# Attention, token mixing and two channel MLPs on one core: block sums in place in PSUM, the first inputs transposed during attention, and later low parts on GpSimd

## The chip, the cores and the metric

The kernel runs on one core of a Trainium2 chip. The metric is the device time in microseconds (us); smaller is better. TensorE is called PE here, VectorE DVE, ScalarE ACT, GpSimd POOL.

## The reference

Inputs are q, k and v of 2 batches x 8 heads x 768 rows x 64. Every row attends to a window of 31 neighbours and to 24 block summaries; then come a token-mixing MLP with a channel MLP, and a layer norm with a second channel MLP. All arithmetic is fp32.

```python
k_sum = k.reshape(B, H, nb, block, D).max(axis=3)
v_sum = v.reshape(B, H, nb, block, D).mean(axis=3)
scores_l_m = np.where(mask_l, scores_l, -1000000000.0)
...
a = np.exp(scores_all)
a = a / (np.sum(a, axis=-1, keepdims=True) + 1e-09)
x = np.matmul(a, v_all)                        # then (2, 768, 512)

h = np.maximum(xt @ w_tok1, 0.0) @ w_tok2      # 768 -> 256 -> 768
u = x + h.transpose(0, 2, 1)
x = u + np.maximum(u @ w_ch1, 0.0) @ w_ch2     # 512 -> 1536 -> 512

xn = (x - mu) / np.sqrt(var + 1e-06) * g_ln
out = x + np.maximum(xn @ w_ch1, 0.0) @ w_ch2  # 512 -> 2048 -> 512
```

## The kernel before

Each fp32 operand of a product is split into a high part (an fp32r copy, made by ACT) and a low part (the value minus its high part, made by DVE or POOL), and a product is three matmuls: low x high, high x low, high x high (`three`, L502).

**Attention** (L619 to L630 on PE) runs over 48 tiles n: scores, transposes of the probabilities, the product with the values. From tile 25 (`MIX0`) on, the token mixing of batch 0 goes between the tiles and ends at tile 42. Behind the loop PE runs the token mixing of batch 1, in which `first_batch` transposes batch 0's rows, eight times three 128x128 transposes; ACT copies each to `raw_in`, POOL makes four sums of blocks of `raw_in` (`t_in`, `sum_inputs`), ACT the high parts of seven inputs (`in_t`, `high_input`), DVE the low parts of two, POOL of the other five (`low_input`).

**The channel MLPs** are 28 pairs q of hidden slices in four groups g (batch 0 and 1 of the first MLP: 6 pairs each; batch 0 and 1 of the second: 8 each). A pair's up product is a 2x2 block product with seven multiplications instead of eight (Strassen-Winograd, `PRODUCTS`, L64). `up(q, i)` is six matmuls of 384 columns into one of two PSUM banks in turn (`up_bank`); between the seven products PE runs the twelve down units (three matmuls of 512 columns each) of the pair before, in the numbers of `DOWNS_AFTER`. The pairs' order on an engine is written out in its `pair`. Products 0 to 3 give p1, u2 and u3; products 4, 5 and 6, with u3 or u2 added by DVE (L1072, L1086, L1099), are three of the four blocks of the hidden layer, written to `c_raw` in SBUF. Of each block ACT makes the ReLU's high part (L828) and DVE the low part (L989). DVE also makes the low parts of the down weights (`low_down`) and of three of the seven up weights (`low_up`), POOL the sums of the up weights (`sum_weights`) and their low parts (`low_sums`, L422).

In 11 of the pairs PE also turns two or three batches (`turn_batch`, L593) of the next group's inputs behind its seven products (`BATCHES_AT`). A product or a batch may only start when the bank that it writes, the one of two products earlier, is free. POOL makes the sums of the next group's inputs in pairs 4, 10 and 17 (`T_AT`), and the last pair of a group (5, 11, 19) starts the next group's `in_t`. The second MLP's layer norm is made by DVE in the first two pairs of groups 1 and 2.

## Time and profile before

| | before |
|---|---|
| median of 3 runs | 644.25 us (643.85 to 644.62) |
| the profiled execution: its time | 643.52 us |
| the profiled execution: its span | 641.7 us |
| mean granted TensorE clock | 0.965 of full |

The span is what the trace covers; the execution's own time is 1.8 us longer. Busy time is what an engine's instructions took; an idle time in brackets in a timeline row is the time that the engine had nothing to run just before the row, and the arrow names what ended it. PEclk is the granted TensorE clock of a stretch, 1.00 being 2.4 GHz and 0.50 being 1.2 GHz.

### The profile page before, as it was taken

The numbers are of one execution on the slowest core, as the hardware profiler recorded it, in microseconds if no ns is written. First come the engines' busy times: TensorE is split into PE (matmuls) and PEld (weight loads), VectorE is DVE, ScalarE is ACT, GpSimd is POOL, SyncE is SP. The second block draws the span as 40 slices with busy tenths as digits, with TensorE's granted clock in tenths as the row PEclk, the third lists the DMA queues.
The fourth block names the chain that finished last, engine by engine and source line by source line (L and its number), as shares of the span: only waits on it lengthen the run. The fifth ranks groups of instructions, "written<-read, shape, count | busy, mean of one in ns | idle before, by whom it ended". The sixth has DMA issues, their size and how long they took to land.

```text
span 641.7 us, 8274 instructions
## 1 busy us (share of the span) xinstructions
PE 592.1 (92%) x2976; PEld 512.1 (80%) x2976; DVE 356.0 (55%) x675; ACT 244.5 (38%) x450; POOL 291.2 (45%) x267
## 2 busy tenths in 40 slices
PE   5989999858999989799989979999899989999998
PEld 2777888647888878688878868888799868989896
DVE  6577665335544548784463878444635664444435
ACT  3577664422333234244423423333324323333321
POOL 5365653274444457534454843444561843333300
PEclk9899999887999989899998979999989989999999
DMA  8977722000311011112110111111101111111302
GB/s 232 243 221 203 213 61 78 0 1 5 121 54 56 30 65 66 65 51 82 65 42 25 66 65 66 67 65 66 65 2 66 66 66 65 66 66 65 132 1 99
DMA packets 24896, 50.34 MB, mean 78 GB/s; under 512 B 7596, under 2 KB 7832, under 8 KB 24856
## 3 DMA queue, kind: packets, MB, share of 16 engines
q1 hardware_dynamic: 24304, 49.37, 23.6%
q10 hardware_dynamic: 552, 0.44, 0.3%
q8 instruction: 24, 0.39, 0.2%
q14 instruction: 16, 0.13, 0.1%
HBM read 46.07 MB, written 3.15 MB: 77 GB/s over the span
## 4 chain that ended last, share of the span: by engine, by line
PE 70%; DVE 13%; POOL 6%; issue 4%; ACT 4%; DMA 2%; SPq 1%; DVEq 0%; POOLq 0%; ACTq 0%
PE bank L500 67%; DVE hidden L989 5%; POOL in_t L453 3%; DVE down_w L914 2%; PE bank L593 2%; DMA tok_stage<-w_tok 1%; ACT hidden L828 1%; ACT in_t L806 1%; DMA k_sb<-k_w 1%; DVE neg_scores L932 1%; DVE c_raw L1086 1%; DVE c_raw L1072 1%; ACT probs L755 1%; DVE k_sb L920 1%; PE bank L535 0%
## 5 line engine op out<-in xcount | busy, mean ns | idle before, releaser
L500 PE MATMUL bank<-down_w,hidden 128*128 128x512 f32 x1008 | 277.1, 404 | 5.3 <-issue 3.1
L500 PEld LDWEIGHTS bank<-down_w,hidden 128*128 128x128 f32 x1008 | 190.0, 193 | 34.0 <-issue 6.6
L500 PE MATMUL bank<-in_t,up_even 128*128 128x384 f32 x588 | 121.9, 344 | 10.7 <-ACT p L834 6.0
L500 PE MATMUL bank<-in_t,up_odd 128*128 128x384 f32 x588 | 123.2, 346 | 7.5 <-DVE c_raw L1086 7.5
L500 PEld LDWEIGHTS bank<-in_t,up_even 128*128 128x128 f32 x588 | 107.4, 192 | 20.5 <-ACT p L834 6.4
L500 PEld LDWEIGHTS bank<-in_t,up_odd 128*128 128x128 f32 x588 | 108.4, 193 | 17.8 <-issue 8.7
L828 ACT ACTIVATE hidden<-c_raw 128x384 fp32r<-128x384 f32 x84 | 44.1, 525 | 176.9 <-DVE c_raw L1072 85.1
L989 DVE SCALAR_TENSOR_TENSOR hidden<-c_raw,hidden 128x384 fp32r<-128x384 f32 x84 | 75.9, 903 | 39.4 <-ACT hidden L828 39.4
L422 POOL TENSOR_TENSOR up_even<-sums_up,up_even 128x1024 fp32r<-128x1024 f32 x14 | 33.6, 2401 | 120.5 <-ACT up_even L818 120.4
L422 POOL TENSOR_TENSOR up_odd<-sums_up,up_odd 128x1024 fp32r<-128x1024 f32 x14 | 33.5, 2392 | 98.5 <-ACT up_odd L818 98.5
L1042 DVE TENSOR_TENSOR u<-bank,p 128x384 f32<-128x384 f32 x28 | 15.6, 557 | 88.3 <-PE bank L500 80.5
L828 ACT ACTIVATE hidden<-bank 128x384 fp32r<-128x384 f32 x28 | 13.8, 492 | 90.9 <-PE bank L500 90.9
L500 PE MATMUL bank<-k_sb,q_sb 128*128 128x364 f32 x96 | 39.1, 493 | 5.6 <-POOL k_sb L371 3.1
L755 ACT ACTIVATE probs<-neg_scores,neg_max 128x182 f32<-128x182 f32 x96 | 37.6, 441 | 13.8 <-DVE neg_max L932 13.2
L932 DVE CUSTOM_DVE_ANT_0 neg_scores<-bank,mask_sb 128x182 f32<-128x182 f32 x96 | 29.3, 342 | 22.8 <-PE bank L500 20.9
L914 DVE TENSOR_TENSOR down_w<-raw_down,down_w 128x1024 fp32r<-128x1024 f32 x28 | 39.5, 1412 | 0.0
L989 DVE SCALAR_TENSOR_TENSOR hidden<-bank,hidden 128x384 fp32r<-128x384 f32 x28 | 15.6, 556 | 34.8 <-ACT hidden L828 34.8
L764 ACT COPY probs_t<-bank 128x384 f32<-128x384 f32 x48 | 22.7, 473 | 30.2 <-PE bank L535 30.0
L1072 DVE TENSOR_TENSOR c_raw<-bank,u 128x384 f32<-128x384 f32 x28 | 15.6, 557 | 29.5 <-PE bank L500 29.2
L414 POOL TENSOR_TENSOR sums_up<-raw_up 128x256 f32<-128x256 f32 x28 | 28.4, 1015 | 2.2
L824 ACT CAST down_w<-raw_down 128x1024 fp32r<-128x1024 f32 x28 | 28.9, 1034 | 0.0
L1059 DVE TENSOR_TENSOR u<-bank,p 128x384 f32<-128x384 f32 x28 | 15.6, 556 | 24.1 <-PE bank L500 24.1
(89 smaller groups left out, 758.4 us busy)
## 6 DMA issues: line engine op xcount, KB each, us to landing
raw_up<-w_ch SPq DMA_DIRECT2D x28, 512.0 KB, 4.3
raw_down<-w_ch SPq DMA_DIRECT2D x28, 512.0 KB, 3.5
k_sb<-k_w SPq DMA_DIRECT2D x16, 273.0 KB, 4.7
v_own<-v_w SPq DMA_DIRECT2D x8, 390.0 KB, 3.1
q_sb<-q_t SPq DMA_DIRECT2D x8, 384.0 KB, 5.7
v_turned<-v_t SPq DMA_DIRECT2D x8, 384.0 KB, 4.3
out<-natural SPq DMA_DIRECT2D x12, 256.0 KB, 3.1
tok_stage<-w_tok SPq DMA_DIRECT2D x4, 384.0 KB, 5.3
```

Source lines behind the costliest of these rows:

```text
L414: tt(sums_up[:, S3], raw[:, A11], raw[:, A21], ALU.subtract).then_inc(up_sum, 1)
L422: nc.gpsimd.tensor_tensor(w[:, 1, 3:7, :], sums_up[:], w[:, 0, 3:7, :].bitcast(F32), ALU.subtract).then_inc(sums_low, 1)
L453: nc.gpsimd.tensor_tensor(in_t[:, i, 1], src, in_t[:, i, 0].bitcast(F32), ALU.subtract).then_inc(in_low_pool, 1)
L500: return nc.tensor.matmul(dst, lhs, rhs, start=start, stop=stop, skip_group_check=True)
L755: nc.scalar.activation(probs[:, n % 2, h * NK:(h + 1) * NK], neg_scores[:, n % 2, h, :], ACT.Exp, bias=neg_max[:, n % 2, h:h + 1], scale=- ...
L764: nc.scalar.copy(probs_t[:, n % 2, :], turn_bank[n % 2][:, 0:3 * P]).then_inc(turned_copied, 1)
L824: nc.scalar.copy(down_w[:, q % 2, :, 0, :], raw_down[:, q % 2]).then_inc(down_high, 1)
L828: nc.scalar.activation(hidden[:, q % 2, f, 0, h * HN:(h + 1) * HN], src, ACT.Relu).then_inc(hid_high, 1)
L914: return nc.vector.tensor_tensor(dst, src, high.bitcast(F32), ALU.subtract)
L932: nc.vector.tensor_tensor_reduce(neg_scores[:, n % 2, h, :], score_bank[n % 3][:, h * NK:(h + 1) * NK], mask_sb[:, kind, (1 - h) * NSUM:(1 ...
L989: nc.vector.scalar_tensor_tensor(out=hidden[:, q % 2, f, 1, at], in0=src, scalar=0.0, in1=hidden[:, q % 2, f, 0, at].bitcast(F32), op0=ALU ...
L1072: nc.vector.tensor_tensor(c_raw[:, 0], product_bank(q, 4)[:, 0:HN], u3[:], ALU.add).then_inc(c_made, 1)
```

## The change

**Block sums.** DVE adds u3 or u2 to products 4, 5 and 6 in the PSUM bank where they stand, and ACT and DVE make the high and low part from the bank. `c_raw` is gone. The bank is free for the next product when the low part is made (`hid_low`), where before it was free when the sum was in `c_raw` (`c_made`). Product 6 no longer accumulates onto product 4; instead DVE adds product 4 to u2 in an instruction of its own. `low_down` moves from between the sum and the low part of block 2 to behind u3; on ACT `high_down` moves ahead of block 1 and `high_sums(q + 1)` behind it.

**First inputs.** Batch 0's 24 transposes are made tile by tile (`first_tile`: four 128x128 transposes into `mix_bank`) in tiles 43 to 47 of attention and once behind the loop; ACT copies 512 columns each time. The four sums and seven low parts of group 0 are DVE's. The up weights of pair 1 are split in pair 0 and no longer in tiles 43 to 45. The first two loads of down weights wait for the last attention tile.

**Later inputs.** The seven low parts of groups 1 to 3 are all POOL's; DVE has none.

The core of the diff:

```diff
@@ DVE, pair(q)
-                dve.wait_ge(u_made, 2 * q + 2)
-                nc.vector.tensor_tensor(c_raw[:, 0], product_bank(q, 4)[:, 0:HN], u3[:], ALU.add).then_inc(c_made, 1)
-                low_hidden(q, 1, c_raw[:, 0])
+                dve.wait_ge(u_made, 3 * q + 2)
+                nc.vector.tensor_tensor(u2[:], product_bank(q, 4)[:, 0:HN], u2[:], ALU.add).then_inc(u_made, 1)
+                add_c(q, 0, 4, u3)
+                low_hidden(q, 1, product_bank(q, 4)[:, 0:HN])
...
+            def add_c(q, k, i, u):
+                c = product_bank(q, i)[:, 0:HN]
+                dve.wait_ge(up_done, 7 * q + i + 1)
+                dve.wait_ge(u_made, 3 * q + 3)
+                nc.vector.tensor_tensor(c, c, u[:], ALU.add).then_inc(c_made, 1)
@@ PE, up and pair(q)
-                                 lambda s: in_t[:, b, s, c, :], i not in (2, 3, 6) and c == 0, c == 1)
+                                 lambda s: in_t[:, b, s, c, :], i not in (2, 3) and c == 0, c == 1)
...
                     if i == 6:
-                        pe.wait_ge(c_made, 3 * q + 1)
+                        pe.wait_ge(hid_low, 4 * q + 2)
...
                     if b < 2:
-                        pe.wait_ge(c_made, 3 * q + 2 + b)
+                        pe.wait_ge(hid_low, 4 * q + 3 + b)
@@ PE, attention
+            def first_tile(t):
+                if t == 0:
+                    pe.wait_ge(u_done, NT)
+                else:
+                    pe.wait_ge(first_copied, t)
+                for c in range(C):
+                    last = nc.tensor.transpose(mix_bank[:, c * P:(c + 1) * P], natural[:, t, c * P:(c + 1) * P],
+                                               ident[:])
+                last.then_inc(first_turned, 1)
...
+                if n >= TURN0:
+                    first_tile(n - TURN0)
@@ ACT, pair(q)
-                if q and q + 1 < NQ:
-                    high_sums(q + 1)
...
                 act.wait_ge(c_made, 3 * q + 1)
-                high_hidden(q, 1, c_raw[:, 0])
-                high_down(q)
+                high_hidden(q, 1, product_bank(q, 4)[:, 0:HN])
+                if making:
+                    high_sums(q + 1)
```

Where the instructions stand, in three places. The first is an ordinary pair on DVE (pair 4 before and after): `up_odd` and `down_w` rows are the low parts of weights, `hidden` rows the low parts of the hidden layer. Before:

```order
L1042 TENSOR_TENSOR u<-bank,p 128x384 [waits p1_copied,up_done]
L914 TENSOR_TENSOR up_odd<-raw_up,up_odd 128x768 [waits up_high]
L989 SCALAR_TENSOR_TENSOR hidden<-bank,hidden 128x384 [waits hid_high]
L1059 TENSOR_TENSOR u<-bank,p 128x384 [waits up_done]
L1072 TENSOR_TENSOR c_raw<-bank,u 128x384 [waits u_made,up_done]
L989 SCALAR_TENSOR_TENSOR hidden<-c_raw,hidden 128x384 [waits hid_high]
L1086 TENSOR_TENSOR c_raw<-bank,u 128x384 [waits up_done]
L914 TENSOR_TENSOR down_w<-raw_down,down_w 128x2x512 [waits down_high]
L989 SCALAR_TENSOR_TENSOR hidden<-c_raw,hidden 128x384 [waits hid_high]
L1099 TENSOR_TENSOR c_raw<-bank,u 128x384 [waits up_done]
L989 SCALAR_TENSOR_TENSOR hidden<-c_raw,hidden 128x384 [waits hid_high]
```

Of the change:

```order
L1061 TENSOR_TENSOR u<-bank,p 128x384 [waits p1_copied,up_done]
L923 TENSOR_TENSOR up_odd<-raw_up,up_odd 128x768 [waits up_high]
L1003 SCALAR_TENSOR_TENSOR hidden<-bank,hidden 128x384 [waits hid_high]
L1080 TENSOR_TENSOR u<-bank,p 128x384 [waits up_done]
L923 TENSOR_TENSOR down_w<-raw_down,down_w 128x2x512 [waits down_high]
L1093 TENSOR_TENSOR u<-bank,u 128x384 [waits u_made,up_done]
L1011 TENSOR_TENSOR bank<-bank,u 128x384 [waits u_made,up_done]
L1003 SCALAR_TENSOR_TENSOR hidden<-bank,hidden 128x384 [waits hid_high]
L1011 TENSOR_TENSOR bank<-bank,u 128x384 [waits u_made,up_done]
L1003 SCALAR_TENSOR_TENSOR hidden<-bank,hidden 128x384 [waits hid_high]
L1011 TENSOR_TENSOR bank<-bank,u 128x384 [waits u_made,up_done]
L1003 SCALAR_TENSOR_TENSOR hidden<-bank,hidden 128x384 [waits hid_high]
```

The low part of `down_w` has moved ahead of the three block sums, the sums write `bank`, every `hidden` row reads `bank`, and one addition (L1093) is new between the product and the first block sum.

The second place is DVE between the end of attention and pair 0: `x_split` is the split of batch 1 for the token mixing, `h_tok` its hidden layer, `t_in` and `in_t` the sums and low parts of the channel MLP's first inputs. Before:

```order
L914 TENSOR_TENSOR up_odd<-raw_up,up_odd 128x768 [waits up_high]
L914 TENSOR_TENSOR x_split<-natural,x_split 128x3x128 [waits x_high_end]
L941 TENSOR_SCALAR den<-bank 128x6 [waits pv_done]
L943 RECIPROCAL den<-den 128x6 [waits den_step]
L945 TENSOR_TENSOR natural<-bank,den 128x3x128 [waits den_step]
L914 TENSOR_TENSOR x_split<-natural,x_split 128x3x128 [waits x_high_end]
L962 SCALAR_TENSOR_TENSOR h_tok<-bank,h_tok 128x512 [waits h_high] x2
L914 TENSOR_TENSOR in_t<-raw_in,in_t 128x768 [waits in_high]
L914 TENSOR_TENSOR in_t<-t_in,in_t 128x768 [waits in_high]
```

Of the change:

```order
L923 TENSOR_TENSOR x_split<-natural,x_split 128x3x128 [waits x_high_end]
L983 TENSOR_TENSOR t_in<-raw_in 128x768 [waits first_copied]
L983 TENSOR_TENSOR t_in<-raw_in,t_in 128x768 [waits first_sum]
L923 TENSOR_TENSOR in_t<-raw_in,in_t 128x768 [waits in_high]
L983 TENSOR_TENSOR t_in<-raw_in 128x768 [waits first_sum]
L923 TENSOR_TENSOR in_t<-t_in,in_t 128x768 [waits in_high]
L971 SCALAR_TENSOR_TENSOR h_tok<-bank,h_tok 128x512 [waits h_high]
L923 TENSOR_TENSOR in_t<-raw_in,in_t 128x768 [waits in_high]
L971 SCALAR_TENSOR_TENSOR h_tok<-bank,h_tok 128x512 [waits h_high]
L923 TENSOR_TENSOR in_t<-t_in,in_t 128x768 [waits in_high]
L983 TENSOR_TENSOR t_in<-raw_in,t_in 128x768 [waits first_sum]
```

The low part of `up_odd` no longer stands ahead of the first `x_split` row; four sums and two more low parts have come to DVE ahead of pair 0, two of them ahead of the first `h_tok` row.

The third place is POOL at the first change of group, from `low_sums` of pair 6 (`up_even`) to the first sum of pair 7's up weights. Before:

```order
L422 TENSOR_TENSOR up_even<-sums_up,up_even 128x1024 [waits up_high,sums_made]
L453 TENSOR_TENSOR in_t<-raw_in,in_t 128x768 [waits in_high,sums_low]
L453 TENSOR_TENSOR in_t<-t_in,in_t 128x768 [waits in_high,in_low_pool] x3
L453 TENSOR_TENSOR in_t<-raw_in,in_t 128x768 [waits in_high,in_low_pool]
L410 TENSOR_TENSOR sums_up<-raw_up 128x256 [waits sums_low,ld_up1,in_low_pool]
```

Of the change:

```order
L424 TENSOR_TENSOR up_even<-sums_up,up_even 128x1024 [waits up_high,sums_made]
L447 TENSOR_TENSOR in_t<-raw_in,in_t 128x768 [waits in_high,sums_low]
L447 TENSOR_TENSOR in_t<-t_in,in_t 128x768 [waits in_high,in_low_pool]
L447 TENSOR_TENSOR in_t<-raw_in,in_t 128x768 [waits in_high,in_low_pool]
L447 TENSOR_TENSOR in_t<-t_in,in_t 128x768 [waits in_high,in_low_pool] x3
L447 TENSOR_TENSOR in_t<-raw_in,in_t 128x768 [waits in_high,in_low_pool]
L412 TENSOR_TENSOR sums_up<-raw_up 128x256 [waits sums_low,ld_up1,in_low_pool]
```

Seven low parts of inputs stand where five stood.

## Rows read from the trace of the kernel before

**Rows 1.** The page, part 1: engine, busy us, share, instructions.

```profile
PE 592.1 (92%) x2976; PEld 512.1 (80%) x2976; DVE 356.0 (55%) x675; ACT 244.5 (38%) x450; POOL 291.2 (45%) x267
```

**Rows 2.** Windows: stretch, length, each engine's busy us, PEclk, DMA share, GB/s.

```profile
113.20:159.50 46.30, 33.57 (x150) 28.71 (x149) 17.30 (x24) 14.55 (x26) 22.33 (x14) 0.85 0.00 0
...
175.90:208.80 32.90, 32.90 (x170) 29.30 (x169) 14.94 (x22) 11.82 (x20) 13.24 (x10) 1.00 0.18 63
...
245.50:272.70 27.20, 22.68 (x103) 19.42 (x102) 21.36 (x27) 8.88 (x14) 18.59 (x14) 0.94 0.22 78
...
332.40:343.30 10.90, 7.85 (x27) 6.48 (x26) 4.46 (x4) 2.76 (x5) 7.71 (x7) 0.69 0.26 96
...
117.00:120.30 3.30, 3.30 (x9) 2.55 (x8) 0.00 (x0) 0.00 (x0) 0.00 (x0) 0.50 0.00 0
```

**Rows 3.** Timeline, 112 to 160 us: start, us, engine, instruction, [idle before <-releaser].

```profile
114.18 2.45 DVE L914 TENSOR_TENSOR x_split<-natural,x_split 128x384 fp32r<-128x384 f32 x1 [0.62 <-ACT x_split L776]
...
116.69 3.91 PE L500 MATMUL bank<-x_split,tok_w 128*128 128x512 f32 x9 [2.96 <-DVE x_split L914]
...
122.81 0.56 DVE L914 TENSOR_TENSOR x_split<-natural,x_split 128x384 fp32r<-128x384 f32 x1 [0.58 <-ACT x_split L776]
...
132.77 0.95 DVE L914 TENSOR_TENSOR in_t<-raw_in,in_t 128x768 fp32r<-128x768 f32 x1
...
133.87 2.12 PE L500 MATMUL bank<-in_t,up_even 128*128 128x384 f32 x6 [3.77 <-DVE in_t L914]
...
146.54 2.29 PE L500 MATMUL bank<-in_t,up_even 128*128 128x384 f32 x6 [6.00 <-ACT p L834]
...
159.54 1.23 PE L500 MATMUL bank<-in_t,up_odd 128*128 128x384 f32 x6
```

**Rows 4.** Timeline of an ordinary pair, 185 to 193 us.

```profile
185.62 0.56 DVE L1072 TENSOR_TENSOR c_raw<-bank,u 128x384 f32<-128x384 f32 x1 [1.18 <-PE bank L500]
...
186.22 0.53 ACT L828 ACTIVATE hidden<-c_raw 128x384 fp32r<-128x384 f32 x1 [2.64 <-DVE c_raw L1072]
...
187.84 1.28 DVE L914 TENSOR_TENSOR down_w<-raw_down,down_w 128x1024 fp32r<-128x1024 f32 x1
...
187.86 1.21 PE L500 MATMUL bank<-in_t,up_even 128*128 128x384 f32 x6
...
190.66 0.55 PE L593 MATMUL bank<-ident,natural 128*128 128x128 f32 x3
...
192.44 1.22 PE L500 MATMUL bank<-in_t,up_odd 128*128 128x384 f32 x6
```

**Rows 5.** Timeline of pair 4, where GpSimd sums the next inputs.

```profile
223.07 2.67 POOL L441 TENSOR_TENSOR t_in<-raw_in 128x768 f32<-128x768 f32 x1
...
224.00 2.15 DVE L989 SCALAR_TENSOR_TENSOR hidden<-c_raw,hidden 128x384 fp32r<-128x384 f32 x1
...
226.68 0.90 PE L593 MATMUL bank<-ident,natural 128*128 128x128 f32 x3 [3.06 <-DVE c_raw L1099]
...
229.78 1.21 PE L500 MATMUL bank<-in_t,up_odd 128*128 128x384 f32 x6
```

**Rows 6.** Timeline around the first change of group.

```profile
249.36 3.79 POOL L453 TENSOR_TENSOR in_t<-t_in,in_t 128x768 fp32r<-128x768 f32 x2 [0.56 <-ACT in_t L806]
...
258.97 1.05 ACT L818 CAST up_odd<-sums_up 128x1024 fp32r<-128x1024 f32 x1 [6.11 <-POOL sums_up L416]
...
264.77 1.28 PE L500 MATMUL bank<-in_t,up_odd 128*128 128x384 f32 x6 [2.73 <-DVE c_raw L1086]
```

**Rows 7.** Instructions of line 989 by operands: duration ns min/median/max, first and last start.

```profile
L989 DVE SCALAR_TENSOR_TENSOR hidden<-c_raw,hidden x84: 543/584/2498, 156.0 to 630.4; 128x384 fp32r<-128x384 f32 x84
L989 DVE SCALAR_TENSOR_TENSOR hidden<-bank,hidden x28: 544/558/560, 149.4 to 621.1; 128x384 fp32r<-128x384 f32 x28
```

**Rows 8.** Waits of TensorE: waiter, releaser, us in total, times, longest us.

```profile
PE bank L593 <- DVE c_raw L1099: 9.1, 3, 3.1
PE bank L500 <- DVE c_raw L1086: 8.4, 5, 2.7
```

More of the change, by code:

```diff
@@ L477, in _ @@
                     sum_weights(1)
[L478 to L482 removed]
+            for q in range(NQ):
                 g, j = group_of(q)
[L484 removed]
+                making = q + 1 < NQ
+                if g and j == 0:
                     for i in range(LATE_IN, 7):
                         low_input(g, i)
[L487 removed]
+                if making and q:
                     sum_weights(q + 1)
+                if making:
                     low_sums(q + 1)
@@ L1047, in pair @@
                     row_stats(g - 1, 5)
[L1048 removed]
+                if q + 1 < NQ:
                     low_up(q + 1)
```

247 lines of the change are left out of this document (122 added, 125 removed).

## The prediction

> **What bounds the kernel now.** First the page: TensorE (PE) is busy for 592.1 us, 92% of the span [rows 1]. So the kernel is bound by PE, and what can be won is of two kinds: time in which PE has nothing to run, and time in which it runs at half clock. The windows show where these lie. In two ordinary pairs (175.9 to 208.8 us) PE is busy for 32.90 of 32.90 us at PEclk 1.00: a pair takes 16.45 us and has no slack to give. From 113.2 to 159.5 us, the hand-over from attention to the first pair of the channel MLP, it is busy for 33.57 of 46.30 us at 0.85; at the first change of group (245.5 to 272.7) for 22.68 of 27.20 us at 0.94 [rows 2].
>
> Then the timeline, for what ends these waits. In the hand-over PE idles 2.96 us until DVE has a low part of `x_split` (2.45 us long, though the same instruction takes 0.56 us at 122.81), 3.77 us for the first low part of `in_t`, and 6.00 us for ACT's copy of p1, which stands on ACT behind the high parts that wait for POOL's four sums [rows 3]. In pair 4 it idles 3.06 us: POOL runs a sum of 2.67 us, DVE's low part of the hidden layer takes 2.15 us beside it, so the sum behind it (L1099) comes late, and the batch at 226.68 waits for that [rows 5]. The trace has the same picture twice more, in pairs 10 and 17: three waits of L593 for L1099 make 9.1 us [rows 8]. By operands, the low part from `c_raw` takes 543 to 2,498 ns, the one from a bank 544 to 560 ns in all 28 cases [rows 7]: with two SBUF operands DVE can be held up by POOL, with one it is not here. At a change of group, five waits for line 1086 cost 8.4 us [rows 8].
>
> After each long idle time PE is granted 1.2 GHz for a while: 9 matmuls at 116.69 take 3.91 us, with PEclk 0.50 [rows 2, 3]; in 332.4 to 343.3 the mean is 0.69 [rows 2]. From the ordinary 1.78 us between the second batch and the next pair (190.66 to 192.44) it becomes 3.10 us behind the wait of pair 4 (226.68 to 229.78), 1.3 us more [rows 4, 5].
>
> **The change, part by part.** I work in the times of the profiled execution (span 641.7 us).
>
> *Hand-over.* The low part of pair 1's up weights on DVE and POOL's low sums leave the end of attention, so `x_split` has its 0.56 us and the wait of 2.96 us goes: PE would be ready at 116.69 - 2.96 = 113.73. Four tiles of four transposes come ahead of it. Three transposes fill a row of 0.55 us with their latency [rows 4]; back to back I take 0.11 us each, so 1.76 us, and ACT's and DVE's split is ready by then. The matmuls start at about 115.4. From 116.69 to the first matmul of pair 1 at 159.54 [rows 3] there are 42.85 us. Without the waits of 3.77 and 6.00 that is 33.1 of work. PEclk 0.85 over 46.30 us means some 14 us at half clock; about 10 of them are busy after 116.69 and would run in half the time, so 28.1 at full clock. 24 transposes leave (2.6), two tiles remain (0.9): 26.4. New waits: the last tile waits for ACT's copy of the one before (0.75, a copy of 512 columns estimated at 0.6); PE then reaches the second layer of batch 1's token mixing about 1.0 us before DVE has its low part, since five sums and low parts at 0.95 us [rows 3] stand ahead of the first `h_tok` row and one between the two; and pair 1 waits about 0.9 us for the bank of product 5 in pair 0, where DVE has extra work. That gives 115.4 + 26.4 + 2.7 = 144.5; I take 144.9. **-14.7 us.** ACT's p1 is then behind one high part that waits for no POOL sum. The loads of down weights start with the end of attention, some 17 us before use.
>
> *Pairs 4, 10 and 17.* `hidden` rows have one SBUF operand and no longer stand beside POOL's sums with two; `low_down`, which still has two, now comes before those sums, since POOL's `low_sums` and with them `sum_inputs` come later. The three waits, 9.1 us [rows 8], go, and the half clock behind them: 1.3 us for the first as above, 1.5 for the third, and up to 2.7 for the second (0.69 over 10.90 us is 6.8 us at half clock, of which some 5.5 busy) [rows 2, 5]. 9.1 + 5.5: **-14.6 us.**
>
> *Every pair: the bank is held longer.* Product 6 now waits until the sum, the high part and the low part of block 0 are made in the bank of product 4. Product 4 is done at 185.62, product 6 starts at 187.86 [rows 4]. New chain: product 4 added to u2 0.56, sum 0.56, high part 0.53 [rows 4], low part 0.56 [rows 7], four hand-overs of 0.04 (ACT starts 0.04 behind the sum's end, rows of pair 2): 2.37, so 187.99. About +0.1 us. Blocks 1 and 2 follow one after the other, because DVE waits for ACT between a sum and its low part: 1.55 to 1.6 us each. The second batch waits for the low part of block 2: 187.99 + 3.1 = 191.1 instead of 190.66 [rows 4], **+0.45 us in each of the 11 pairs with batches**. Against it stands that `low_down` (1.28 us at 187.84 [rows 4]) no longer lies between these steps; it now lies behind u3, where DVE idled 1.18 us before 185.62 [rows 4]; overlapping its neighbours' ends a little, it is just covered. If that cover is missed, the whole chain is late by as much. In the some 13 ordinary pairs without batches only the 0.1 remains: the next pair begins two down units later. 11 x 0.45 + 13 x 0.1 = **+6.2 us**.
>
> No row has DVE writing to PSUM from PSUM. Lower bound: the sum from a bank to SBUF, 0.56 us; upper: the slowest row of the same width, 2.15 us beside POOL [rows 5], which would not hold here as the sum has one SBUF operand. I take 0.56, as it is the same operation, and widen the range by 0.1 us for each of three sums in the 11 pairs, 3 us.
>
> The Trainium skill speaks against reading the bank: in "VectorE: DVE Perf Modes", section on the TRN2 errata, an instruction of VectorE with a PSUM source has a fixed part of 120 cycles at 0.96 GHz, one with an SBUF source 58, so 65 ns more for each low part, or an estimated 2 us more over 11 chains of three. The trace does not agree: 558 ns from a bank against 543 at least and 584 in the median from `c_raw` [rows 7]. The sum above goes by the trace.
>
> *Changes of group.* Before, the first costs 4.5 us of idle time and, at a mean of 0.94 over 27.2 us, 1.6 us of clock [rows 2]; with short waits for L1086 in the pair behind it (part of the 8.4 us [rows 8]) I count 6.8 us, and take the other two as equal. After, `low_sums` stands behind the high part of block 0 and ends about 6 us later, and POOL has seven low parts of 1.9 us (3.79 for two [rows 6]) behind it, of which the new group's first product needs one. I find the next group's first product about 2.5 us late; product 6 of that pair 1.6 us late, as `low_down` meets POOL's low parts and add-outs stand ahead of the block sums; and the sums of pair 7's weights end about 5 us later than the 258.97 of before, where ACT waited 6.11 us for them [rows 6]. That wait no longer stands ahead of block 0's high part but ahead of block 1's, and I find 0.75 us for it and 0.4 for the product behind, where it cost 2.73 us and more [rows 6]. With 0.5 us for short waits that is 5.8 us, against 6.8: **-1.0 us each, -3**; half clock behind the wait of 2.5 us would add some 1.4 each.
>
> Sum: 641.7 - 14.7 - 14.6 + 6.2 - 3.0 = 615.6 us of span. The execution's own time is 1.8 us above its span, 617.4, and the median of the runs is 0.7 above this execution: **618 us**.
>
> **The rivals.**
> - *The hand-over gives half* (0.15): DVE now has 11 sums and low parts there at 0.95 us each, 10.5 us; if ACT and DVE hand over less well than one after the other, or PE drops to half clock once more, 7 us are lost again: 625 us. For it: PE's largest waits were of this kind. Against: POOL is idle then, so nothing holds DVE up.
> - *POOL alone is too slow at the changes of group* (0.12): the low parts meet DVE's two-operand rows at 2.5 us instead of 1.9, and PE is granted half clock behind each wait. 3 to 4 us for each: 628 us. For it: POOL already had the critical chain there. Against: two fewer DVE rows with two SBUF operands.
> - *The waits of pairs 4, 10 and 17 stay* (0.08): the change doesn't do what it says, because another row with two SBUF operands, `low_down`, is held by POOL's sums. Three waits of 3 us and the clock come back: 632 us. Against: by the order they no longer meet.
> - *Slower than before* (0.05): holding the bank is what decides. The chain has three sums in place; in 11 pairs all three lie before the second batch, in the others one or two before a product. If a sum in place takes x longer, that is about 60x over the program. From x = 0.45 us on (1.0 us a sum) it eats the gain of 26; at 0.5 us, 648 us. For it: no row shows this form. Against: every narrow bank row is within 0.56.
> - The forecast has 0.60; its own range is 612 to 625 us.
>
> **How the numbers follow.** Below: a hand-over with fewer of the new waits and changes of group without half clock, 609. Above, up to 631, which takes in the first two rivals and leaves the last two, and the forecast's own tails, outside. A measurement of this kernel can tell about 0.2% (1.3 us). Slower: the last rival, 0.05, and 0.01 for several at once; same 0.02; faster the rest.
>
> **What would show it.** In the changed kernel's trace: the first matmul of pair 1 at about 145 us; no wait of 3 us in pairs 4, 10, 17, but one of about 0.4 us in front of each second batch, ended by a `hidden` row; `bank<-bank,u` at about 0.56 us; `hidden` rows never over 0.6 us; in the first change of group a wait of 2 to 3 us for POOL's `in_t`. The prediction is wrong if sums in place are longer, if the second batch waits for over 1 us, or if the half clock returns in the hand-over.

## The result, and the profile after

The changed kernel takes 620.25 us (median of 4 runs, 618.54 to 621.6) against 644.05 us (643.22 to 644.62): ratio 0.963, 95% interval 0.9597 to 0.9663. The forecast was 618 us, range 609 to 631. The profiled execution took 621.6 us, its span is 619.8.

The page of the changed kernel, its first part and its largest DVE groups (columns as in [rows 1]; then line, engine, operation, out<-in, shapes, count | busy us, mean ns | idle before it in us and what ended it):

```profile
PE 589.4 (95%) x2976; PEld 499.5 (81%) x2976; DVE 339.7 (55%) x706; ACT 243.2 (39%) x448; POOL 267.8 (43%) x264
...
L1003 DVE SCALAR_TENSOR_TENSOR hidden<-bank,hidden 128x384 fp32r<-128x384 f32 x112 | 62.5, 558 | 82.3 <-ACT hidden L835 82.3
L1011 DVE TENSOR_TENSOR bank<-bank,u 128x384 f32<-128x384 f32 x84 | 46.9, 559 | 2.9
```

PE's share rose from 92 to 95% [rows 1]: PE stands idle for 30.4 us of the span where it stood idle for 49.6, so nearly all of the gain is idle time. The sum in place, for which no row stood before, takes 559 ns, and no low part is held any more: 112 of them average 558 ns, where 84 from `c_raw` reached 2,498 [rows 7].

Windows of the changed kernel: the hand-over, most of two ordinary pairs (3 and 4), and the stretch behind a change of group.

```profile
112.50:143.80 31.30, 29.00 (x158) 25.16 (x156) 23.20 (x37) 15.77 (x27) 1.84 (x1) 1.00 0.24 84
176.90:210.10 33.20, 33.05 (x165) 28.41 (x163) 14.76 (x24) 11.66 (x20) 9.98 (x10) 1.00 0.17 64
230.80:234.20 3.40, 3.40 (x11) 2.93 (x10) 0.00 (x0) 1.88 (x3) 3.24 (x3) 0.50 0.00 0
```

The hand-over of [rows 2], 46.30 us at 0.85, has become 31.30 us at 1.00. The ordinary pairs, which had no idle time before, now have a little. Behind attention, half clock is left only where GpSimd (POOL) is late, behind the first and third change of group. The timeline of the changed kernel: hand-over, ordinary pair, first change of group.

```profile
114.29 0.56 DVE L923 TENSOR_TENSOR x_split<-natural,x_split 128x384 fp32r<-128x384 f32 x1 [0.87 <-ACT x_split L770]
...
119.52 0.63 PE L586 MATMUL bank<-ident,natural 128*128 128x128 f32 x4 [0.77 <-ACT raw_in L780]
...
128.45 1.62 PE L492 MATMUL bank<-h_tok,tok_w 128*128 128x512 f32 x6 [1.07 <-DVE h_tok L971]
...
187.65 0.56 DVE L1093 TENSOR_TENSOR u<-bank,u 128x384 f32<-128x384 f32 x1
188.15 1.23 PE L492 MATMUL bank<-in_t,up_odd 128*128 128x384 f32 x6
188.31 0.57 DVE L1011 TENSOR_TENSOR bank<-bank,u 128x384 f32<-128x384 f32 x1
189.44 0.56 DVE L1003 SCALAR_TENSOR_TENSOR hidden<-bank,hidden 128x384 fp32r<-128x384 f32 x1 [0.56 <-ACT hidden L835]
190.05 1.32 PE L492 MATMUL bank<-in_t,up_odd 128*128 128x384 f32 x6
192.61 0.56 DVE L1003 SCALAR_TENSOR_TENSOR hidden<-bank,hidden 128x384 fp32r<-128x384 f32 x1 [0.56 <-ACT hidden L835]
193.22 0.55 PE L595 MATMUL bank<-ident,natural 128*128 128x128 f32 x3
...
225.94 2.41 POOL L424 TENSOR_TENSOR up_even<-sums_up,up_even 128x1024 fp32r<-128x1024 f32 x1 [4.52 <-ACT up_even L825]
228.43 1.81 POOL L447 TENSOR_TENSOR in_t<-raw_in,in_t 128x768 fp32r<-128x768 f32 x1
230.38 1.90 PE L492 MATMUL bank<-in_t,up_even 128*128 128x384 f32 x6 [2.15 <-POOL in_t L447]
...
241.09 2.34 DVE L923 TENSOR_TENSOR down_w<-raw_down,down_w 128x1024 fp32r<-128x1024 f32 x1
```

Three things answer to the rows of before. The low part of `x_split` takes 0.56 us where it took 2.45, and the waits of 2.96, 3.77 and 6.00 us [rows 3] are now 0.77 and 1.07. The chain in the bank (187.65 to 190.05) is the one that the prediction wrote out; product 6 (190.05) and the pair's second batch (193.22) start just behind the low part that frees their bank. And the new group's first product waits 2.15 us for POOL, which first makes a low part of weights (225.94) although it had stood idle for 4.52 us.

### The profile page after: what moved, and what is told of

It is laid out like the page before. It is cut to its first block, busy times and chain, and to the rows that moved or that the text cites. A ratio compares the mean times of both kernels' runs of the same rounds, so it can differ in the third digit from the quotient of the medians.

```text
span 619.8 us, 8385 instructions
## 1 busy us (share of the span) xinstructions
PE 589.4 (95%) x2976; PEld 499.5 (81%) x2976; DVE 339.7 (55%) x706; ACT 243.2 (39%) x448; POOL 267.8 (43%) x264
## 4 chain that ended last, share of the span: by engine, by line
PE 66%; DVE 14%; ACT 7%; issue 6%; POOL 3%; DMA 2%; SPq 1%; DVEq 0%; POOLq 0%; ACTq 0%
PE bank L492 63%; DVE bank L1011 4%; ACT hidden L835 4%; POOL in_t L447 3%; DVE hidden L1003 2%; DVE u L1093 2%; PE bank L595 1%; DMA tok_stage<-w_tok 1%; DVE to_turn L1048 1%; DMA k_sb<-k_w 1%; DVE in_t L923 1%; ACT in_t L813 1%; DVE neg_scores L941 1%; DVE k_sb L929 1%; ACT probs L749 1%
## 5 line engine op out<-in xcount | busy, mean ns | idle before, releaser
L492 PE MATMUL bank<-down_w,hidden 128*128 128x512 f32 x1008 | 273.4, 399 | 0.0
L492 PEld LDWEIGHTS bank<-down_w,hidden 128*128 128x128 f32 x1008 | 187.4, 190 | 27.2
L835 ACT ACTIVATE hidden<-bank 128x384 fp32r<-128x384 f32 x112 | 55.1, 492 | 258.0 <-DVE bank L1011 158.3
L492 PEld LDWEIGHTS bank<-in_t,up_even 128*128 128x128 f32 x588 | 104.7, 189 | 26.4 <-issue 10.5
L492 PEld LDWEIGHTS bank<-in_t,up_odd 128*128 128x128 f32 x588 | 104.4, 188 | 16.9 <-DVE hidden L1003 6.1
L1003 DVE SCALAR_TENSOR_TENSOR hidden<-bank,hidden 128x384 fp32r<-128x384 f32 x112 | 62.5, 558 | 82.3 <-ACT hidden L835 82.3
L424 POOL TENSOR_TENSOR up_odd<-sums_up,up_odd 128x1024 fp32r<-128x1024 f32 x14 | 33.6, 2398 | 135.4 <-ACT up_odd L825 135.4
L424 POOL TENSOR_TENSOR up_even<-sums_up,up_even 128x1024 fp32r<-128x1024 f32 x14 | 34.2, 2441 | 124.0 <-ACT up_even L825 123.9
L1011 DVE TENSOR_TENSOR bank<-bank,u 128x384 f32<-128x384 f32 x84 | 46.9, 559 | 2.9
L749 ACT ACTIVATE probs<-neg_scores,neg_max 128x182 f32<-128x182 f32 x96 | 37.7, 441 | 15.9 <-DVE neg_max L941 15.3
L843 ACT COPY p<-bank 128x384 f32<-128x384 f32 x28 | 13.4, 480 | 36.5 <-PE bank L492 36.4
L492 PE MATMUL bank<-v_own,probs_t 128*128 128x65 f32 x192 | 26.7, 261 | 0.0
L412 POOL TENSOR_TENSOR sums_up<-raw_up 128x256 f32<-128x256 f32 x28 | 24.1, 860 | 4.0 <-POOL up_odd L424 1.9
```

What stands on the lines that cost most here:

```text
L412: tt(sums_up[:, S1], raw[:, A21], raw[:, A22], ALU.add).then_inc(up_sum, 1)
L424: nc.gpsimd.tensor_tensor(w[:, 1, 3:7, :], sums_up[:], w[:, 0, 3:7, :].bitcast(F32), ALU.subtract).then_inc(sums_low, 1)
L492: return nc.tensor.matmul(dst, lhs, rhs, start=start, stop=stop, skip_group_check=True)
L749: nc.scalar.activation(probs[:, n % 2, h * NK:(h + 1) * NK], neg_scores[:, n % 2, h, :], ACT.Exp, bias=neg_max[:, n % 2, h:h + 1], scale=- ...
L835: nc.scalar.activation(hidden[:, q % 2, f, 0, h * HN:(h + 1) * HN], src, ACT.Relu).then_inc(hid_high, 1)
L1003: nc.vector.scalar_tensor_tensor(out=hidden[:, q % 2, f, 1, at], in0=src, scalar=0.0, in1=hidden[:, q % 2, f, 0, at].bitcast(F32), op0=ALU ...
```

## The experiments

Medians are of 4 to 6 runs each, the range or the 95% interval in brackets; the kernel before took 643.37 us beside the first four, 644.53 beside the next four, 643.55, 644.65 and 644.3 beside the last. Times of a pair run from its first matmul to the next pair's, in the timeline. A profile is of one execution: the first matmul of pair 0 lies anywhere between 125.75 and 129.07 us in the thirteen kernels with the new attention part, which is the same in all, so two spans can differ by 3 us without a cause in the pairs. Blocks 1 to 3 of the hidden layer are those of products 4, 5 and 6, as in the section on the change; the prediction counts them from 0.

### The parts of the change

**The hand-over alone**: before, with the attention part of the change (`first_tile`, group 0's sums and low parts on DVE, down loads later); `c_raw`, the old order and the later groups as before.

```diff
+                if n >= TURN0:
+                    first_tile(n - TURN0)
```

> The kernel before with the hand-over part alone: batch 0's transposes in attention tiles 43 to 47, DVE's four sums and seven low parts for group 0, pair 1's up weights split in pair 0; block sums in c_raw and the split of later low parts (two DVE, five GpSimd) as before. By my theory the parts add up, and this one gives what the first matmul of pair 1 shows (159.5 to 143.8 us): 15.7 us less than before, 628 us, with the waits of 3 us in pairs 4, 10 and 17 and at the changes of group where they were. The rival, that part of the 15.7 us is only borrowed and given back in the pairs behind (weights split later, loads later), gives 632 us or more.

629.21 us, ratio 0.9769 (0.9738 to 0.9799): -14.2 us. The three waits for L1014, the sum for the second batch, are all there (9.0 us in total). So the hand-over is worth 14 us by itself, close to the 15.7 of the theory, little of it is given back in the pairs behind (the rival's 632 us), and the waits of pairs 4, 10 and 17 are another matter.

**The later low parts on POOL, too**: the seven low parts of groups 1 to 3, otherwise as the kernel above.

```diff
-                    for i in range(DVE_IN, LATE_IN):
+                    for i in range(LATE_IN):
                         low_input(g + 1, i)
```

> As e1, and all seven low parts of groups 1 to 3 on GpSimd; sums in c_raw, old order of the weights' work. By my theory GpSimd carries the chain at each change of group, and two more low parts of 1.9 us in front of its sums of weights cost 2 to 4 us each time: 634 to 640 us. The rival, that GpSimd has room and the move costs nothing, gives 628 us.

633.44 us (629.01 to 636.27), ratio 0.983 (0.9776 to 0.9884): about 4 us slower than without this part, and just below the forecast 634 to 640. The two intervals touch, so that it costs by itself is likely, not shown. Pairs 6, 12 and 20 take 21.1, 21.2 and 20.5 us, where they took 19.3, 19.3 and 18.7; pairs 7, 13 and 21 give back 0.9, 0.3 and 2.7.

**The order, but not the bank**: the changed kernel with the block sums written to `c_raw` again, the bank free at the sum, and product 6 accumulated onto product 4 again, without the addition to u2.

```diff
-                nc.vector.tensor_tensor(c, c, u[:], ALU.add).then_inc(c_made, 1)
+                nc.vector.tensor_tensor(c_raw[:, k], c, u[:], ALU.add).then_inc(c_made, 1)
```

> The changed kernel, but block sums go to c_raw and the bank is free at the sum, as before; everything else (hand-over, GpSimd's low parts, the new places of low_down, high_down and high_sums) as changed. Theory: the second SBUF operand is what cost the 3 us waits, so low parts from c_raw again take up to 2.5 us beside GpSimd's sums, and waits of 2 to 3 us stand in or behind pairs 4, 10 and 17, while the ordinary pairs with batches fall from 17.05 back to about 16.5 us: the two about cancel, 618 to 623 us. Rival: the new order alone takes the waits away, then this kernel is faster than the changed one by the price of the held bank, about 9 us: 611 us.

622.51 us (622.08 to 624.29), ratio 0.9679 (0.9658 to 0.9701). The sum is inside the range, but its reasons were wrong: pairs with batches take 17.0 us, not 16.5, and pairs 4, 10 and 17 take 17.0, 17.0 and 17.1, without any wait of 3 us. The timeline of this kernel, of an ordinary pair, of pair 4 (208.21) and behind the first change of group:

```profile
190.56 2.39 POOL L425 TENSOR_TENSOR up_even<-sums_up,up_even 128x1024 fp32r<-128x1024 f32 x1 [11.04 <-ACT up_even L826]
...
191.22 2.15 DVE L1004 SCALAR_TENSOR_TENSOR hidden<-c_raw,hidden 128x384 fp32r<-128x384 f32 x1 [0.59 <-ACT hidden L836]
...
193.29 0.55 DVE L1012 TENSOR_TENSOR c_raw<-bank,u 128x384 f32<-128x384 f32 x1
...
193.89 0.55 PE L596 MATMUL bank<-ident,natural 128*128 128x128 f32 x3 [0.37 <-DVE c_raw L1012]
...
208.21 2.16 DVE L1004 SCALAR_TENSOR_TENSOR hidden<-c_raw,hidden 128x384 fp32r<-128x384 f32 x1 [0.59 <-ACT hidden L836]
...
248.71 2.37 POOL L425 TENSOR_TENSOR up_odd<-sums_up,up_odd 128x1024 fp32r<-128x1024 f32 x1 [1.23 <-ACT up_odd L826]
249.13 2.36 DVE L1004 SCALAR_TENSOR_TENSOR hidden<-c_raw,hidden 128x384 fp32r<-128x384 f32 x1 [0.59 <-ACT hidden L836]
...
251.59 2.88 PE L493 MATMUL bank<-down_w,hidden 128*128 128x512 f32 x6 [1.61 <-issue]
```

With two SBUF operands the low part is still held, now beside POOL's low part of the weights: 1116 ns in the mean of 84. In an ordinary pair PE waits 0.37 us for it in front of the second batch, and the pair takes as long (17.0 us) as with the held bank of the changed kernel. Behind the changes of group it costs a wait and half clock: pairs 7, 13 and 21 take 19.3, 21.7 and 19.7 us, against 16.6, 16.7 and 16.0; pairs 6, 12 and 20 give back 1.4, 2.2 and 1.2.

**The bank, but not the order**: the changed kernel with `low_down` between sum and low part of block 2, and `high_sums`, `high_down` and two of each later group's `high_input` on ACT where they were.

```diff
-                low_down(q)
...
                 add_c(q, 1, 5, u3)
+                low_down(q)
                 low_hidden(q, 2, product_bank(q, 5)[:, 0:HN])
```

> The changed kernel with sums in place, but low_down between the sum and the low part of block 2, high_sums ahead of block 0's high part and high_down behind it, as before. Theory: the order matters where GpSimd is busy: low_down (two SBUF operands) is blocked beside GpSimd's sums in pairs 4, 10 and 17, ACT's high parts wait for the sums of weights at a change of group, and in every pair 1.3 us of low_down lie in the chain that holds the bank, so a batch pair takes about 18 us: 635 us or more. Rival: in place sums alone bring the gain and the order is worth under 3 us: 623 us at most.

627.2 us (626.18 to 628.27), ratio 0.9747 (0.9725 to 0.9769), between the two theories (635 or more, 623 at most). Pairs with batches take 17.7 us, pairs 4, 10 and 17 take 19.0, 18.9 and 19.0: in pair 4 `low_down` takes 2.67 us at 211.17, beside POOL's sums of inputs, and the two batches behind wait 1.50 and 0.34 us. The four medians with the hand-over and POOL's low parts together:

| | `c_raw` | in the bank |
|---|---|---|
| old order | 633.4 | 627.2 |
| new order | 622.5 | 620.3 |

The order is worth 10.9 us with `c_raw` and 6.9 us with the bank; the bank is worth 6.2 and 2.3 us. The second is hardly more than the intervals, and the changed kernel was timed apart from the other three, with 644.05 us for the kernel before beside it. The waits of 3 us of [rows 5] go by either, but with the bank alone pairs 4, 10 and 17 stay 1.3 us longer than their neighbours.

### What the change left

**One low part back on DVE**: that of each later group's first product.

```diff
+                if ending:
+                    low_first(0, g + 1)
```

> The changed kernel with the first low part of each later group's inputs (product 0's own) back on VectorE, ahead of the sum of block 2 in the last pair of the group before; the other six stay on GpSimd. In the changed kernel product 0 of groups 1 to 3 waits 2.15, 2.15 and 2.16 us for that low part on GpSimd (L447), and TensorE runs at half clock for 3.4 us after two of the three waits, which costs about 1.7 us each. Theory A (the waits come from GpSimd alone, which takes the low part only behind its own low part of the sums' weights, L424): the three waits go, of each some 0.3 to 0.5 us comes back because the sums of blocks 2 and 3 stand 0.95 us later on VectorE; with the half clock gone 620.3 - 3 x 1.7 - 2 x 1.7 = about 612, range 610 to 615. Rival B (VectorE's low part reads two SBUF operands while GpSimd is at L424 and is held to its end, as low_down was for 2.34 us): it takes about 2.4 us instead of 0.95, blocks 2 and 3 are late by as much, product 0 or 1 waits 1 to 2 us for hidden; 616 to 620.

614.92 us (614.3 to 615.62), ratio 0.9541 (0.9522 to 0.956): 5.3 us less than the changed kernel. That is in theory A's range (610 to 615), at its upper end. DVE's low part starts at 225.93, 0.57 us before POOL's low part of the weights, and takes 0.95 us; PE stands idle for 0.11 us in front of product 0, and no half clock is left between 25 and 610 us. So giving POOL this low part, in the order of the change, did not pay.

**POOL's first two low parts ahead of its low part of the weights**, in the last pair of each group, into the 4.52 us in which it stood idle.

```diff
+                if ending:
+                    low_input(g + 1, 0)
+                    low_input(g + 1, 1)
                 if making:
                     low_sums(q + 1)
```

> The changed kernel with GpSimd's first two low parts of the next group's inputs put ahead of the low part of the sums' weights (L424) in the last pair of each group; nothing else moves. In the changed kernel GpSimd sits idle there from 221.4 to 225.9 us, while the high parts of these two inputs are ready at 220.4 and 221.1. Theory A: the waits of 2.15, 2.15 and 2.16 us at product 0 and the half clock behind two of them (about 1.7 us each) go, and nothing else comes: 620.3 - 6.5 - 3.4 = 610.4, range 609 to 613. Rival B: the two low parts last past 225.9 (2.4 us each beside VectorE), L424 ends 1 us later and product 1 or 3, which need the sums' low parts, wait in its place: 613 to 617. Rival C (waits of a pair are covered by another one right behind): over 617.

612.01 us (611.16 to 614.47), ratio 0.9506 (0.9484 to 0.9528), -8.2 us: three waits and two stretches of half clock, as theory A has it. It is the order on POOL, not its speed, that made them. Behind it, product 6 of pair 6 waits 1.57 us for `hidden`, 1.46 in the changed kernel.

**One down unit from the end of each pair to just ahead of product 6.**

```diff
-DOWNS_AFTER = {0: (2, 2, 2, 2, 1, 1, 2), 2: (2, 2, 1, 1, 1, 1, 1, 1, 2), 3: (2, 1, 1, 1, 1, 1, 1, 1, 1, 2)}
+DOWNS_AFTER = {0: (2, 2, 2, 2, 1, 2, 1), 2: (2, 2, 1, 1, 1, 2, 1, 1, 1), 3: (2, 1, 1, 1, 1, 2, 1, 1, 1, 1)}
```

> The changed kernel with one down unit (0.70 us of TensorE) moved from the end of each pair to just ahead of product 6, in all pairs but none of the sums changed. In the changed kernel product 6 starts 0.14 us late in the ordinary pairs and batch 2 about 0.29 us late, both behind hidden L1003, since the product's bank is held until its low part is read. Theory A (the in-place sums hold a bank too long by just that): pairs with batches fall from 17.05 to about 16.6, pairs without from 16.0 to about 15.85, and the changes of group gain some of their waits of 0.9 to 1.5 us for hidden: 620.3 - 14 x 0.43 - 8 x 0.14 - 2 = about 611, range 609 to 614. Rival B (the +0.6 and +0.3 us per pair are matmuls that run slower, not waits): 617 to 620. Rival C (with one unit less at the end of a pair the next pair's products 0 and 1 wait for the last low part or for the copied batch): 620 or more.

616.92 us (614.3 to 619.66), ratio 0.9571 (0.9547 to 0.9595): -3.3 us by the medians, just below B's range (617 to 620) and far from A's (609 to 614). Pairs without batches fall from 16.0 to 15.75 us, those with batches from 17.05 to 16.7: the first had waited for the bank only; in the others the second batch still starts up to 0.2 us late. The changes of group gained little: at the first, product 6 of pair 6 waits 0.42 us instead of 1.46, but pair 7's first product, one unit earlier now, 1.66 instead of 0.16.

**Both.**

> The two edits before together (GpSimd's two low parts ahead, one down unit ahead of product 6). If both theories A hold and the gains add: 620.3 - 9.9 - 9 = about 602, range 600 to 606. If the second of them is nothing: 610 to 612. If neither: 617 to 621.

607.46 us (606.17 to 608.02), ratio 0.9417 (0.9397 to 0.9437): the gains add, 12.8 us against 8.2 and 3.3. The forecast of 600 to 606 had taken theory A's larger gain for the down unit, and is missed.

**Both, with `c_raw`.** The same edit as for the order without the bank.

> The kernel of the two edits together (607.46 us), with the block sums written to c_raw in SBUF again and the bank free at the sum; the order, GpSimd's share and the unit ahead of product 6 stay. Theory A (a low part that reads c_raw beside a running GpSimd operation is held for as long as that one lasts, as at 249.13 in the run with c_raw and the new order, 2.36 us instead of 0.56, which made TensorE wait 1.61 us and then run 3.4 us at half clock): behind each change of group a held low part costs 1.6 to 3.3 us, the bank free earlier gives back a part of the waits of 1.2 and 0.9 us for hidden in the pair before; 607.5 + 3 x 2.5 - 3 x 1.5 = about 610, range 608 to 613. Rival B (with the order right the sums in place earn nothing, and the bank is held for nothing): 603 to 607.

606.14 us (604.31 to 607.74), ratio 0.9401 (0.9364 to 0.9437). Rival B: once the order is right, on POOL too and with the unit ahead of product 6, sums in place earn nothing in total that can be told. By pairs both theories are half right. With batches `c_raw` gives 16.4 us against 16.7; pairs 6, 12 and 20 take 17.0, 16.7 and 15.7 against 18.3, 18.3 and 16.6; pairs 7, 13 and 21 take 20.2, 20.0 and 18.3 against 16.6, 16.7 and 15.9.

**Both, with `low_down` later** in the first pair of groups 1 to 3, behind the low part of block 1.

```diff
+                if not opening:
+                    low_down(q)
...
                 low_hidden(q, 1, product_bank(q, 4)[:, 0:HN])
+                if opening:
+                    low_down(q)
```

> The kernel of the two edits together (607.46 us), with the low part of the down weights (low_down, two SBUF operands) in the first pair of groups 1 to 3 moved from between u3 and the sums to behind the low part of block 1; all other pairs as before. In that kernel it takes 2.80 us at 237.05, beside GpSimd's last low part of the inputs (L447 at 236.92), against 1.22 us in an ordinary pair, and product 6 then waits 1.22 us and the next pair's product 0 another 0.86 us, both for hidden. Theory A (these waits are the held low_down, 2.8 us ahead of the chain of sums): in each of the three pairs 1.2 to 2.1 us go; 607.5 - 3 x 1.5 = about 603, range 601.5 to 605. Rival B (the output's additions and row statistics, 2 x 1.28 us per product in that chain, are enough to keep it late, or low_down is held by GpSimd at its new place too): 605.5 to 608.

606.95 us (605.14 to 608.81), ratio 0.9416 (0.9381 to 0.945): no gain that can be told, rival B. The timeline of this kernel in pair 6:

```profile
243.23 1.22 DVE L927 TENSOR_TENSOR down_w<-raw_down,down_w 128x1024 fp32r<-128x1024 f32 x1
243.29 1.75 POOL L418 TENSOR_TENSOR sums_up<-raw_up,sums_up 128x256 f32<-128x256 f32 x1
...
245.08 1.05 ACT L829 CAST up_odd<-sums_up 128x1024 fp32r<-128x1024 f32 x1 [2.35 <-POOL sums_up L418]
245.56 0.55 DVE L1015 TENSOR_TENSOR bank<-bank,u 128x384 f32<-128x384 f32 x1
...
246.14 0.49 ACT L839 ACTIVATE hidden<-bank 128x384 fp32r<-128x384 f32 x1
...
247.37 1.30 PE L496 MATMUL bank<-in_t,up_odd 128*128 128x384 f32 x6 [1.54 <-DVE hidden L1007]
```

`low_down` now takes 1.22 us, but it started first, so POOL's sum was held (1.75 us instead of 0.74), and ACT waits for that sum in front of its cast. The wait of PE before product 6 is gone, the one before pair 7 is 1.54 us where it was 0.86. Two chains end together there: ACT's cast is done at 246.13, and block 2's sum, which stands on DVE behind `low_down`, an addition of the output and a row's statistics, at 246.11. So either would have kept the high part of block 2 (246.14) as late, and this run does not tell them apart.

**One block in place, in six pairs**: both edits, `c_raw`, and the sum of block 2 in the bank in the last pair of groups 0 to 2 and the first of groups 1 to 3.

```diff
+        def sum_at(q, k):
+            return product_bank(q, 5)[:, 0:HN] if k == 1 and in_place(q) else c_raw[:, k]
```

> The kernel of the two edits with c_raw in SBUF (606.14 us), with one block sum in place in PSUM again: that of block 2 (product 5's bank), in the last pair of groups 0 to 2 and the first pair of groups 1 to 3 alone, six of 84 sums. With c_raw its low part starts beside GpSimd's low part of the sums' weights (L425) there and takes 2.76 and 2.44 us instead of 0.56; TensorE then waits 1.01 and 2.58 us in front of the down matmuls, and 3.4 us of half clock stand behind the second at two of three places. In the other pairs c_raw lets go of the bank at the sum: 16.4 and 15.8 us a pair, where the sums in place take 16.7 and 15.8. Theory A (a sum in place pays only where its low part meets a long operation on GpSimd, and costs a late batch elsewhere): pairs 7, 13 and 21 fall from 20.2, 20.0 and 18.3 to some 17.0, 16.9 and 16.0, the pairs ahead of them lose up to 0.4: 606.1 - 8.6 + 1 = about 598, range 596.5 to 600. Rival B (something else of these pairs, so the low parts of blocks 1 and 3 from c_raw, or the held bank, is late in its place): 601 to 607.

604.17 us (602.54 to 605.49), ratio 0.9373 (0.9343 to 0.9404), 2 us less than with `c_raw` alone, within the intervals. Pairs 7, 13 and 21 fall to 17.4, 17.4 and 15.9, but pairs 6, 12 and 20 rise to 18.5, 18.3 and 16.8: rival B, another row is late. The timeline of this kernel:

```profile
237.28 2.73 POOL L456 TENSOR_TENSOR in_t<-raw_in,in_t 128x768 fp32r<-128x768 f32 x1
...
243.49 1.04 ACT L840 CAST up_odd<-sums_up 128x1024 fp32r<-128x1024 f32 x1 [2.99 <-POOL sums_up L427]
244.44 0.48 ACT L850 ACTIVATE hidden<-bank 128x384 fp32r<-128x384 f32 x1
...
244.96 0.56 DVE L1018 SCALAR_TENSOR_TENSOR hidden<-bank,hidden 128x384 fp32r<-128x384 f32 x1 [2.06 <-ACT hidden L850]
...
245.66 2.16 PE L505 MATMUL bank<-in_t,up_odd 128*128 128x384 f32 x6 [2.55 <-DVE hidden L1018]
```

Block 2's sum was in the bank at 242.90, but ACT stood for 2.99 us in front of a cast that waits for POOL's sums of weights, and its high part of block 2 is queued behind. POOL is late with the sums: the low parts of inputs lie ahead of them, the last one (237.28) held to 2.73 us by `low_down`.

**That cast one block later**, in the first pair of groups 1 to 3, with block 3 of the six pairs in the bank too.

```diff
-                if making:
+                if making and not opening:
                     high_sums(q + 1)
...
                 high_hidden(q, 2, sum_at(q, 1))
+                if making and opening:
+                    high_sums(q + 1)
```

> The mixed kernel (604.17 us) with ScalarE's high part of the sums' weights (L840, high_sums) in the first pair of groups 1 to 3 moved behind the high part of block 2, and block 3's sum of the same six pairs in place too, since GpSimd's low part of the sums' weights will then lie beside its low part. In the mixed kernel ScalarE stands 2.99 us in front of that cast, until GpSimd, late with the last low part of the inputs (237.28 to 240.01), has made the sums at 243.46; the high part of block 2 stands behind it in ScalarE's order, and the next pair's product 0 waits 2.55 us, with 3.4 us of half clock behind two of the three. Theory A (the wait is ScalarE's order, behind GpSimd's queue): each of the three waits goes but for 0.3 us, the half clock too; 604.2 - 3 x 2.2 - 2 x 1.7 = about 594, and 596 if the sums' low part is late for product 1 once; range 593 to 598. Rival B (the output's additions and row statistics between the sums on VectorE, 1.28 us per product, make blocks 2 and 3 nearly as late, as in the kernel with all sums in place): 599 to 603.

597.84 us (596.06 to 598.66), ratio 0.9288 (0.9253 to 0.9322): theory A, at the upper end of its range. The timeline of this kernel, the same place:

```profile
241.01 0.49 ACT L852 ACTIVATE hidden<-bank 128x384 fp32r<-128x384 f32 x1 [2.44 <-DVE bank L1031]
...
241.58 1.05 ACT L842 CAST up_odd<-sums_up 128x1024 fp32r<-128x1024 f32 x1
242.24 1.30 PE L505 MATMUL bank<-in_t,up_odd 128*128 128x384 f32 x6 [0.64 <-DVE hidden L1023]
...
245.22 0.97 PE L505 MATMUL bank<-in_t,up_odd 128*128 128x384 f32 x4 [0.28 <-POOL up_odd L433]
```

The wait of 2.55 us is 0.64, no stretch between 25 and 590 us is at half clock, and a change of group (pairs 5 to 7) takes 49.0 us, where it took 54.4 in the changed kernel and 54.6 before. This version beats both kernels: 22 us below the change, 46 below before. The run moved two things at once, the cast and block 3's sum; the waits of ACT that went are the cast's, but how the 6.3 us divide between the two was not measured.

## Why the prediction was right, step by step

By the profiled executions the span fell from 641.7 to 619.8 us, -21.9; forecast was -26.1. The terms, from the pairs' starts in both timelines:

| term | forecast | measured |
|---|---|---|
| hand-over | -14.7 | -15.7 |
| pairs 4, 10, 17, with the half clock behind them | -14.6 | -14.9 |
| bank held, 11 pairs with batches | +5.0 | +7.5 |
| the same, pairs without | +1.3 | +2.3 |
| changes of group | -3.0 | -2.3 |
| last matmul to the end | 0 | +1.2 |

The second row takes pairs 4, 10, 17 and 18 and 1.2 us of pair 11, which was at half clock before; what the held bank costs in these pairs is in the third and fourth. The first row holds whatever the two executions differ by in attention, and the start of pair 0 alone varies by 3 us between them, so its 1.0 us beyond the forecast tells nothing.

- **Hand-over: right.** The first matmul of pair 1 is at 143.8 us (forecast 144.9, 0.4 of it added to the sum without a reason; 159.54 before [rows 3]). The three new waits, forecast 0.75, 1.0 and 0.9, are 0.77, 1.07 and 0.47, and no half clock is left. The run with this part alone gives 14.2 of the 23.8 us between the medians.
- **Pairs 4, 10 and 17: size right, reason too narrow.** The three waits of 9.1 us [rows 8] are gone and the pairs take 17.0, 17.0 and 17.1. The step said that the low part's single SBUF operand does this, together with the place of `low_down`. The run with `c_raw` in the new order has no such wait either: there the low part at 208.21 is held as long as before (2.16 us, now by POOL's low part of the weights), and the batch behind waits 0.40 us. What the step did not write down is the `low_down` of before, just ahead of [rows 5] in the timeline:

```profile
219.61 1.68 DVE L989 SCALAR_TENSOR_TENSOR hidden<-c_raw,hidden 128x384 fp32r<-128x384 f32 x1 [0.59 <-ACT hidden L828]
...
221.68 2.40 DVE L914 TENSOR_TENSOR down_w<-raw_down,down_w 128x1024 fp32r<-128x1024 f32 x1
```

  Three held instructions (1.68, 2.40 and 2.15 us) stood one behind the other ahead of the sum that frees the bank; in the run with `c_raw` the new order takes the longest out and leaves one. The bank with the old order takes 0.9 to 2.2 us off these pairs (against `c_raw` in the old order) and no more, since `low_down` stays in the chain.
- **Bank held: mis-sized, the step that failed.** The mechanism is as forecast: product 6 starts at 190.05, 0.14 us late, the second batch at 193.22, some 0.3 us late, and a low part in the bank is never held. But a pair with batches costs 0.6 us more than before, not 0.45, and one without 0.3, not 0.1 (of these there are 7, and not some 13: nine others stand at the changes of group). The chain itself was well sized: 2.37 us from product 4's end to product 6, measured 2.40 (187.65 to 190.05). By the starts of the matmuls, pair 3 lost 0.13 us before product 6, 0.28 before the second batch, and two things that the step had not counted: product 6 takes 1.32 us behind its wait, where product 5 takes 1.23 and an unwaited one 1.22, and the down matmuls follow one another at 0.234 instead of 0.230 us, 0.09 in all. The last is there with `c_raw` in the new order too, so it is not the bank's. Moving one down unit took 0.25 us off the pairs without batches, the wait and the longer product. In pairs 8 and 14 the cost is 1.0 us each, not seen ahead: the layer norm's `to_turn`, in the same DVE queue, takes 1.94 us for two at 266.22 beside POOL's L424 and the POOL sum behind it, where two at 263.72 took 1.00, and the next product 0.76 us of waiting for `hidden`. These make 3.5 of the 4.2 us by which the span was missed.
- **Sum in place 0.56 us: right** (559 ns). The range for it was not needed, nor was the rival that ends slower, which wanted 1.0 us.
- **Changes of group: right in sum and place, by waits.** Forecast 2.5 us for the first product, 1.6 and 0.75 for those behind; measured 2.15, 1.46 and 0.16 at the first; `low_down` meets POOL's low parts as forecast, 2.34 us at 241.09. The prediction took POOL's order there as given; that wait and its half clock were worth 8 us.
- **The end**: the trace ends 4.3 us after the last matmul (3.2 before); over all kernels it is 3.2 to 4.3, and no run here tells why.
- **Luck.** The profiled execution is 4.2 us above its forecast (621.6 against 617.4), the median 2.25 us (620.25 against 618): the forecast put the median 0.7 us above the profiled execution, as before, and it came out 1.35 below. That took back half of the miss.

The rule quoted in the prediction, 120 cycles for a PSUM source against 58, shows in no row: the shortest low part takes 543 ns from `c_raw` and 544 from the bank [rows 7]. The same section of the Trainium skill ("VectorE: DVE Perf Modes", on the TRN2 errata) gives (N + 151) cycles at 0.96 GHz for an fp32 addition, an estimated 557 ns at 384 columns, and that agrees with 559.

Still open: why the second batch remains 0.2 us late in the pairs with batches when a unit more lies ahead of it. The chain of three in-place blocks, 1.6 us each, is the likely reason, as those pairs lose it with `c_raw`; a chain made shorter was not tried.

## What to carry to other kernels

Before moving an operand to PSUM to escape GpSimd, see whether the held instruction can stand elsewhere: here the order was worth 7 to 11 us, the bank 2 to 6, and once GpSimd's order and the down units were right too, nothing in total. In the fastest kernel the bank is kept only in the six pairs where the low part meets a long GpSimd instruction. Holding a bank until its last reader costs little if a unit of other work lies ahead of the next product (16.0 us a pair against 15.75). When a wait survives the repair of its nearest cause, follow the releasers across every in-order queue: the last 6 us here came when ScalarE no longer stood in front of a cast that GpSimd was not ready for (together with one more sum in place).

## What the runs showed of the hardware

- A DVE instruction with two SBUF operands that starts beside a POOL instruction is held to about its end: POOL 248.71 + 2.37 = 251.08, DVE's low part ended at 249.13 + 2.36 = 251.49, so 0.41 us later, where an unheld one takes 0.56 in all. It goes the other way round too: 1.75 us for a POOL sum that met `low_down` (0.74 otherwise). The Trainium skill says so in "SBUF — State Buffer", section "Who interferes with whom": a lock for the whole instruction, and the order of issue decides who blocks. The traces agree in both directions.
- `to_turn`, with one wide SBUF operand, was held as well (1.94 us for two, beside L424 and a sum): "one SBUF operand" was no protection for this operation.
- The first block sum waits for L1093, whose operand it overwrites, and started 0.10 us after its end (187.65 + 0.56 to 188.31); a DVE instruction that waits for nothing starts some 0.09 us before the one ahead ends (189.44 + 0.56 to 189.91).
- The length of the last wait alone does not tell whether TensorE falls to 1.2 GHz: behind 2.15 us it did at two of three changes of group (PEclk 0.50 from 230.80 to 234.20), behind 2.40 us, with one down unit moved, it did not at the first, behind 1.57 us it stayed at 2.4 GHz with POOL's low parts ahead, and behind 1.61 us it fell with `c_raw` in the new order (six down matmuls in 2.88 us instead of 1.56).
